# Blocks and token sums split in the order of their use, a third token sum on VectorE, and TensorE's waits moved into the first F pair

## The chip, the cores and the metric

One Trainium2 chip; the program runs on one of its cores. The metric is the device time of one execution in microseconds, the median of several runs. TensorE, VectorE (DVE in the profile), ScalarE (ACT), GpSimd (POOL) and SyncE (SP, which issues the DMAs here) each work through a list of instructions of their own and wait for one another by semaphores.

## The reference

Three stages: a sparse attention (2 batches of 8 heads, 768 tokens, head size 64), a mixture of 4 experts that every token passes, and a routed mixture of 8 experts. The change lies in the second one:

```python
def _moe_ref(x, domain_probs, w1, w2):      # x: 1536 x 512
    p = domain_probs / (domain_probs.sum(-1, keepdims=True) + 1e-09)
    out = np.zeros((N, D), dtype=np.float32)
    for e in range(4):                      # w1: 512 x 1024, w2: 1024 x 512
        h = np.maximum(x @ w1[e], 0.0)
        out += p[:, e:e + 1] * (h @ w2[e])
    return out
```

## The kernel before

**High and low parts.** A float32 product is made of three matmuls on a high part (rounded by ScalarE) and a low part (the rest, subtracted by VectorE): high x high, high x low, low x high. So each weight and each activation is split before TensorE can use it: ScalarE writes `..._hi`, then VectorE writes `..._lo`.

**The order of the mixture.** Expert 0 runs for all four groups of 384 tokens along with the attention (`group_steps`, c = 0 to 3). Then come five *passes* (`PASSES`): experts 1, 2, 3 on batch 0, then experts 1 and 2 on batch 1; pass 3 (`SWITCH`) is the first of batch 1. Expert 3 on batch 1 is done after them in the plain way, as c = 4 and 5 of `group_steps` (c = G is the first of these two).

**A pass.** Its first layer (`factors`) is a block multiplication in seven products instead of eight. w1 is cut into 2 x 2 blocks; three of them are used as they are (A11, A12, A22), the fourth arrives in the place of S4 and is overwritten by it. S1 to S4 are sums of blocks, T1 to T4 sums of the halves of x. For each of four F pairs i TensorE makes the products in the order A12, S1·T1, A11, A22·T4, S2·T2, S4, S3·T3, six matmuls of 128x384 each (`block`, lines 2000 to 2002). ScalarE takes products out of PSUM (`put`), VectorE adds a second product to them (`join`, line 1362), and both split the result into `hb_hi` and `hb_lo`. The second layer (`rows_out`) makes six row tiles of 24 matmuls of 128x512 on PSUM banks 2 and 3 in turn; VectorE adds each to `acc` (`add_more`, line 1377), and row tile tt waits for the addition of tile tt - 2. For expert 0 that addition is `add_rows`, line 1224.

**The preparation of the next pass.** SyncE loads four blocks (`load_blocks`) when the pass before has made its last product. VectorE makes S1 to S4 in place (`block_sums`, lines 1336 to 1344), ScalarE rounds all seven blocks in `BLOCK_ORDER` (`high_blocks`, line 953), VectorE makes the low parts (`low_blocks`, line 1350, 128x1024 each). VectorE does this between the additions of the row tiles. When the batch changes (before pass 0 and before pass 3) the token sums come too: T1, T2 and T4 on VectorE (lines 1308 to 1324, three, two and two subtractions or additions of 128x768), T3 on GpSimd (`third_sum`, lines 758 to 762); ScalarE rounds them (`high_sums`, line 964), VectorE makes their low parts (`low_sums`, line 1329). Before pass 3 SyncE brings back the half of x that was set aside (`x_back`).

**What TensorE waits for.** Ahead of a pass it waits for all seven low blocks of the pass and, in passes 0 and 3, for all four low sums:

```python
pe.wait_ge(acc_ok, 2 + GR * G)
for t in range(len(PASSES)):
    pe.wait_ge(block_ok, BLOCKS * (t + 1))
    if t in (0, SWITCH):
        pe.wait_ge(t_ok, 4 * (PASSES[t][0] + 1))
    factors(t, route_fill if t == SWITCH else lambda k: None)
```

The wait for `acc_ok` stands ahead of the loop and is for the last addition of expert 0. After the last pass TensorE waits for `rows_added` of all 30 row tiles and, in c = G, for all four low pieces of w1 (`w1_ok`), of which VectorE makes the last one (`low_w1`, line 1206) after the last row addition. During pass 3 TensorE also transposes finished rows for the router (`route_turn`, line 1939), which wait for `rows_added` of the first three passes.

Of the kernel before, what the change touches and what calls it, by code (L numbers as in the profile page):

```python
# [18 lines left out]
def sparse_attention_moe_moe(nc, q, k, v, dprobs, w1, w2, w_skip, w_gate, v1, v2, out):  # L19
# [60 lines left out]
    BLOCK_ORDER = (A22, A11, S1, A12, S3, S2, S4)  # L80
    T1, T2, T3, T4 = range(4)
    T_ORDER = (T1, T2, T4, T3)
# [36 lines left out]
    with ExitStack() as ctx:  # L119
# [296 lines left out]
        def _(sp):  # L416
# [251 lines left out]
        def _(gp):  # L668
# [80 lines left out]
            def third_sum(b):  # L749

                (b12, b12_lo), (b22, b22_lo) = x_block(0, 1), x_block(1, 1)
                to = halves(t_sum_at(b, T3))
                if b:
                    gp.wait_ge(x_back, 32)
                else:
                    gp.wait_ge(x_saved, 32)
                    gp.wait_ge(l1_done, FC * G)
                nc.gpsimd.tensor_tensor(to, b22, b12, ALU.subtract).then_inc(t_pool, 1)
                gp.wait_ge(t_pool, 3 * b + 1)
                nc.gpsimd.tensor_tensor(to, to, b22_lo, ALU.add).then_inc(t_pool, 1)  # L760
                gp.wait_ge(t_pool, 3 * b + 2)
                nc.gpsimd.tensor_tensor(to, to, b12_lo, ALU.subtract).then_inc(t_pool, 1)

            for b in range(B):
                third_sum(b)

# [56 lines left out]
        def _(act):  # L823
# [121 lines left out]

            def high_blocks(t):

                for k, j in enumerate(BLOCK_ORDER):
                    if j in (A22, A11, A12):
                        act.wait_ge(block_sent[(A22, S4, A11, A12).index(j)], 16 * (t + 1))  # L950
                    else:
                        act.wait_ge(block_sum, 4 * t + (S1, S3, S2, S4).index(j) + 1)
                    nc.scalar.activation(block_part(wb_hi, j), block_in(j), ACT.Copy).then_inc(block_hi_ok, 1)

            def high_sums(b):

                for k, j in enumerate(T_ORDER):
                    if j == T3:
                        act.wait_ge(t_pool, 3 * (b + 1))
                    else:  # L960
# [1284 lines left out]
```

## Time and profile before

| | |
|---|---|
| median of 3 runs | 753.19 us (750.95 to 754.45) |
| the profiled execution's own time | 749.69 us |
| its span | 748.0 us |
| TensorE busy | 711.6 us (95%) |
| TensorE weight loads | 587.3 us (79%) |
| VectorE busy | 430.7 us (58%) |
| ScalarE busy | 291.5 us (39%) |
| GpSimd busy | 83.7 us (11%) |
| TensorE's mean granted clock | 0.990 |

Times in the profile count from the first instruction of the span. Matmuls overlap, so a matmul's duration is longer than the distance from its start to the next one's, and a group's busy time says less about TensorE than its pauses. A wait for several semaphores is put down to the one that came last. In the chain of waits each piece begins where the piece before it ended; a run of the same instruction is one piece (x3, x4).

### The profile page before, as it was taken

The numbers are of one execution on the slowest core, as the hardware profiler recorded it, in microseconds if no ns is written. First come the engines' busy times: TensorE is split into PE (matmuls) and PEld (weight loads), VectorE is DVE, ScalarE is ACT, GpSimd is POOL, SyncE is SP. The second block draws the span as 40 slices with busy tenths as digits, with TensorE's granted clock in tenths as the row PEclk, the third lists the DMA queues.
The fourth block names the chain that finished last, engine by engine and source line by source line (L and its number), as shares of the span: only waits on it lengthen the run. The fifth ranks groups of instructions, "written<-read, shape, count | busy, mean of one in ns | idle before, by whom it ended". The sixth has DMA issues, their size and how long they took to land.

```text
span 748.0 us, 12356 instructions
## 1 busy us (share of the span) xinstructions
PE 711.6 (95%) x4530; PEld 587.3 (79%) x4531; DVE 430.7 (58%) x1055; ACT 291.5 (39%) x651; POOL 83.7 (11%) x103
## 2 busy tenths in 40 slices
PE   5699999999979999999997899999989999999997
PEld 4588898988869889989985898899888986444454
DVE  4987665453976745773769459756543154544341
ACT  4654454451516605533641356055122211533330
POOL 2611000000400000000012000200000003432321
PEclk9999999999999999999999999999999999999999
DMA  9894722213423303303070733033215269599900
GB/s 205 214 207 91 155 61 56 51 28 95 186 85 112 113 1 114 109 4 113 3 279 1 253 113 113 1 113 113 84 60 195 85 222 373 202 398 395 391 18 21
DMA packets 88239, 101.60 MB, mean 136 GB/s; under 512 B 54616, under 2 KB 54892, under 8 KB 87280
## 3 DMA queue, kind: packets, MB, share of 16 engines
q1 hardware_dynamic: 85520, 96.14, 40.0%
q0 software_dynamic: 2656, 4.66, 2.0%
q8 instruction: 35, 0.57, 0.3%
q14 instruction: 28, 0.23, 0.1%
HBM read 88.32 MB, written 12.96 MB: 135 GB/s over the span
## 4 chain that ended last, share of the span: by engine, by line
PE 77%; DVE 13%; DMA 6%; issue 2%; SPq 1%; ACT 1%; POOL 0%; DVEq 0%; POOLq 0%
PE ps L1757 14%; PE ps L1759 13%; PE ps L1758 13%; PE ps L2000 7%; PE ps L2001 6%; PE ps L2002 6%; PE ps L2153 4%; PE ps L2125 4%; DMA sets<-in_moe_w 3%; DVE wb_lo L1350 3%; DMA xt_lo<-x_aside 2%; PE ps L1819 2%; PE ps L1791 2%; PE ps L1950 1%; PE ps L1805 1%
## 5 line engine op out<-in xcount | busy, mean ns | idle before, releaser
L2000 PE MATMUL ps<-xt_hi,wb_hi 128*128 128x384 f32 x280 | 94.7, 338 | 6.0 <-DVE acc L1224 3.9
L2002 PE MATMUL ps<-xt_hi,wb_lo 128*128 128x384 f32 x280 | 94.3, 337 | 0.0
L2001 PE MATMUL ps<-xt_lo,wb_hi 128*128 128x384 f32 x280 | 94.3, 337 | 0.0
L969 ACT ACTIVATE h_raw<-ps 128x384 f32<-128x384 f32 x80 | 39.3, 491 | 105.8 <-PE ps L2002 103.8
L1758 PE MATMUL ps<-v_lo_acc,hb_hi 128*128 128x512 f32 x180 | 70.6, 392 | 0.0
L1757 PE MATMUL ps<-xt_hi,w_hi 128*128 128x384 f32 x188 | 65.6, 349 | 2.4 <-issue 2.1
L1362 DVE TENSOR_TENSOR h_raw<-ps,h_raw 128x384 f32<-128x384 f32 x80 | 41.3, 552 | 42.9 <-PE ps L2002 42.9
L1759 PE MATMUL ps<-xt_hi,w_lo 128*128 128x384 f32 x188 | 63.1, 336 | 0.0
L1758 PE MATMUL ps<-xt_lo,w_hi 128*128 128x384 f32 x188 | 63.0, 335 | 0.0
L907 ACT ACTIVATE h_hi<-ps 128x384 fp32r<-128x384 f32 x48 | 23.6, 492 | 97.1 <-PE ps L1759 96.9
L1757 PE MATMUL ps<-w_hi,h_hi 128*128 128x512 f32 x144 | 58.2, 404 | 0.4 <-DVE acc L1224 0.4
L2000 PEld LDWEIGHTS ps<-xt_hi,wb_hi 128*128 128x128 f32 x280 | 53.1, 190 | 6.9 <-issue 6.8
L975 ACT ACTIVATE hb_hi<-h_raw 128x384 fp32r<-128x384 f32 x80 | 40.8, 525 | 43.2 <-DVE h_raw L1362 43.1
L1759 PE MATMUL ps<-w_hi,h_lo 128*128 128x512 f32 x144 | 56.4, 391 | 0.0
L1758 PE MATMUL ps<-w_lo,h_hi 128*128 128x512 f32 x144 | 56.2, 390 | 0.0
L2001 PEld LDWEIGHTS ps<-xt_lo,wb_hi 128*128 128x128 f32 x280 | 53.0, 189 | 0.1
L2125 PE MATMUL ps<-sets,acc 128*64 128x512 f32 x224 | 51.6, 599 | 1.6 <-DVE sets L1698 0.6
L2002 PEld LDWEIGHTS ps<-xt_hi,wb_lo 128*128 128x128 f32 x280 | 53.1, 189 | 0.0
L1757 PE MATMUL ps<-v_hi_first,hb_hi 128*128 128x512 f32 x120 | 47.6, 396 | 5.1 <-DVE acc L1377 5.1
L2153 PE MATMUL ps<-sets,acc 128*64 128x256 f32 x448 | 51.6, 382 | 0.7 <-ACT acc L1059 0.7
L1377 DVE SCALAR_TENSOR_TENSOR acc<-ps,dp,acc 128x512 f32<-128x512 f32 x30 | 22.5, 749 | 48.4 <-PE ps L1759 48.4
L1367 DVE SCALAR_TENSOR_TENSOR hb_lo<-h_raw,hb_hi 128x384 fp32r<-128x384 f32 x80 | 42.1, 554 | 12.0 <-ACT hb_hi L975 11.8
(262 smaller groups left out, 1400.1 us busy)
## 6 DMA issues: line engine op xcount, KB each, us to landing
sets<-in_moe_w SPq DMA_DIRECT2D x72, 512.0 KB, 7.8
w_raw<-in_moe_w SPq DMA_DIRECT2D x20, 512.0 KB, 6.1
acc<-in_moe_w SPq DMA_DIRECT2D x10, 768.0 KB, 5.3
stage<-in_moe_w SPq DMA_DIRECT2D x8, 512.0 KB, 4.5
stage<-in_k SPq DMA_DIRECT2D x16, 192.0 KB, 4.7
acc<-in_v SPq DMA_DIRECT2D x4, 768.0 KB, 6.4
x_rows<-acc SPq DMA_DIRECT2D x4, 768.0 KB, 6.0
out_rows<-acc SPq DMA_DIRECT2D x4, 768.0 KB, 7.6
```

The source lines that it names most:

```text
L969: nc.scalar.activation(h_raw[:, f, half * GT:(half + 1) * GT], ps[:, bank, 0:GT], ACT.Copy).then_inc(put_by, 1)
L975: nc.scalar.activation(hb_hi[cols], h_raw[cols], ACT.Relu).then_inc(hb_hi_ok, 1)
L1362: TT(to, ps[:, bank, 0:GT], to, ALU.add).then_inc(joined, 1)
L1367: nc.vector.scalar_tensor_tensor(out=hb_lo[cols], in0=h_raw[cols], scalar=0.0, in1=hb_hi[cols].bitcast(F32), op0=ALU.max, op1=ALU.subtract ...
L1757: mm(dst, a_hi, b_hi, start=start, stop=False)
L1758: mm(dst, a_hi, b_lo, start=False, stop=False)
L1759: return mm(dst, a_lo, b_hi, start=False, stop=stop)
L2000: mm(to, wb_hi[w], hi(c), start=(c == 0 and not onto), stop=False, skip_group_check=onto)
L2001: mm(to, wb_hi[w], lo(c), start=False, stop=False, skip_group_check=onto)
L2002: last = mm(to, wb_lo[w], hi(c), start=False, stop=(c == HALF_D - 1), skip_group_check=onto)
L2125: last = mm(ps[j * QT:(j + 1) * QT, 0, 0:FQ], xt2[:, from_c:from_c + QT], wset[:, 0, at:at + FQ], start=(c == 0), stop=(c == KC - 1))
L2153: last = mm(ps[j * QT:(j + 1) * QT, bank, 0:DQ], ht2[:, at:at + QT], wset[:, 0, to:to + DQ], start=(f == 0), stop=(f == FC - 1))
```

## The change

`BLOCK_ORDER` and `T_ORDER` become the order in which the products use them, and the split of a token sum follows that of the block it is used with (`T_AFTER`), on ScalarE, on VectorE and in TensorE's waits. SyncE loads the four blocks in another order. The wait for the low parts goes from ahead of the pass into `block`, where each of the seven products of the first F pair waits for its own. `third_sum` moves from GpSimd to VectorE: before pass 0 it stands ahead of the low blocks, before pass 3 after row tile 3's addition. Between the row tiles of pass 2, VectorE's work is put in a new order (`between`); in pass 3 the last four low blocks go behind the fifth addition. In c = G the first product is made as all high-weight matmuls, then the low ones, each waiting for its piece, and the wait for `rows_added` goes behind the first layer.

```diff
-    BLOCK_ORDER = (A22, A11, S1, A12, S3, S2, S4)
+    BLOCK_ORDER = (A12, S1, A11, A22, S2, S4, S3)
...
-    T_ORDER = (T1, T2, T4, T3)
+    T_ORDER = (T1, T4, T2, T3)
+    T_AFTER = {S1: T1, A22: T4, S2: T2, S3: T3}
...
-                for k, (to, row, col) in enumerate(((A22, 1, 1), (S4, 0, 1), (A11, 0, 0), (A12, 1, 0))):
+                for k, (to, row, col) in enumerate(((A12, 1, 0), (S4, 0, 1), (A22, 1, 1), (A11, 0, 0))):
...
             def high_blocks(t):
+                for j in BLOCK_ORDER:
+                    high_block(t, j)
+                    if t in (0, SWITCH) and j in T_AFTER:
+                        high_sum(PASSES[t][0], T_AFTER[j])
...
+            def third_sum(b):
+                (b12, b12_lo), (b22, b22_lo) = x_block(0, 1), x_block(1, 1)
+                to = halves(t_sum_at(b, T3))
+                if b == 0:
+                    dve.wait_ge(x_saved, 32)
+                    dve.wait_ge(l1_done, FC * G)
+                follow(TT(to, b22, b12, ALU.subtract))
+                follow(TT(to, to, b22_lo, ALU.add))
+                TT(to, to, b12_lo, ALU.subtract).then_inc(t_sum, 1)
...
-            low_blocks(0, range(3))
+            third_sum(0)
+            low_blocks(0, range(2))
             add_rows(c, 0, c, 0, True)
-            low_blocks(0, range(3, BLOCKS))
+            low_blocks(0, range(2, 4))
             add_rows(c, 0, c, 1, True)
-            low_sums(0)
+            low_blocks(0, range(4, BLOCKS))
             add_rows(c, 0, c, 2, True)
...
+                if t + 1 == SWITCH:
+                    if tt == 0:
+                        block_sums(t + 1, 0)
+                        block_sums(t + 1, 1)
+                    if tt == 1:
+                        low_blocks(t + 1, range(1))
+                    if tt == 2:
+                        first_sum(1)
+                        second_sum(1)
+                    if tt == 3:
+                        fourth_sum(1)
+                        third_sum(1)
+                    if tt == 4:
+                        low_blocks(t + 1, range(1, 4))
+                    if tt == 5:
+                        low_blocks(t + 1, range(4, BLOCKS))
+                    return
...
+                elif c == G:
+
+                    pe.wait_ge(joined, 4 * FP * len(PASSES))
+                    pe.wait_ge(h_ok, FC * c + 1)
+                    for kc in range(KC):
+                        pe.wait_ge(w1_hi_ok, PIECES * e + kc + 1)
+                        mm(ps[:, 0, 0:GT], w1_hi[:, kc, 0:P], xt_hi[:, kc, 0:GT], start=(kc == 0), stop=False)
+                        mm(ps[:, 0, 0:GT], w1_hi[:, kc, 0:P], xt_lo[:, kc, 0:GT], start=False, stop=False)
+                    for kc in range(KC):
+                        pe.wait_ge(w1_ok, PIECES * e + kc + 1)
+                        last = mm(ps[:, 0, 0:GT], w1_lo[:, kc, 0:P], xt_hi[:, kc, 0:GT], start=False, stop=(kc == KC - 1))
...
+                if c == G:
+                    pe.wait_ge(rows_added, TPH * len(PASSES))
...
-            def block(j, i, moving, bank, onto=False):
+            def block(t, j, i, moving, bank, onto=False):
 
                 hi, lo = moving
+                if i == 0:
+                    pe.wait_ge(block_ok, BLOCKS * t + BLOCK_ORDER.index(j) + 1)
+                    if t in (0, SWITCH) and j in T_AFTER:
+                        pe.wait_ge(t_ok, 4 * PASSES[t][0] + T_ORDER.index(T_AFTER[j]) + 1)
...
             for t in range(len(PASSES)):
-                pe.wait_ge(block_ok, BLOCKS * (t + 1))
-                if t in (0, SWITCH):
-                    pe.wait_ge(t_ok, 4 * (PASSES[t][0] + 1))
                 factors(t, route_fill if t == SWITCH else lambda k: None)
...
-            pe.wait_ge(rows_added, TPH * len(PASSES))
```

The change moves instructions at three places. First VectorE in front of pass 0, from the low blocks to the last addition of expert 0 (`wb_lo` is a low block, `xt_lo` a low token sum, `acc` a row addition). Before:

```order
L1350 TENSOR_TENSOR wb_lo<-w_raw,wb_hi 128x1024 [waits block_hi_ok] x3
L1224 TENSOR_SCALAR acc<-ps,dp 128x512 [waits l2_done]
L1350 TENSOR_TENSOR wb_lo<-w_raw,wb_hi 128x1024 [waits block_hi_ok] x4
L1224 TENSOR_SCALAR acc<-ps,dp 128x512 [waits l2_done]
L1329 TENSOR_TENSOR xt_lo<-t_raw,xt_hi 128x768 [waits t_hi_ok] x2
L1329 TENSOR_TENSOR xt_lo<-h_rows,xt_hi 128x768 [waits t_hi_ok]
L1329 TENSOR_TENSOR xt_lo<-x_raw,xt_hi 128x768 [waits t_hi_ok]
L1224 TENSOR_SCALAR acc<-ps,dp 128x512 [waits l2_done]
```

With the change, whose lines are those of the changed program, from the last step of the third sum (`x_raw`) on:

```order
L1316 TENSOR_TENSOR x_raw<-x_raw,xt_lo 128x768 [waits t_step]
L1341 TENSOR_TENSOR wb_lo<-w_raw,wb_hi 128x1024 [waits block_hi_ok] x2
L1320 TENSOR_TENSOR xt_lo<-t_raw,xt_hi 128x768 [waits t_hi_ok]
L1206 TENSOR_SCALAR acc<-ps,dp 128x512 [waits l2_done]
L1341 TENSOR_TENSOR wb_lo<-w_raw,wb_hi 128x1024 [waits block_hi_ok] x2
L1320 TENSOR_TENSOR xt_lo<-h_rows,xt_hi 128x768 [waits t_hi_ok]
L1206 TENSOR_SCALAR acc<-ps,dp 128x512 [waits l2_done]
L1341 TENSOR_TENSOR wb_lo<-w_raw,wb_hi 128x1024 [waits block_hi_ok]
L1320 TENSOR_TENSOR xt_lo<-t_raw,xt_hi 128x768 [waits t_hi_ok]
L1341 TENSOR_TENSOR wb_lo<-w_raw,wb_hi 128x1024 [waits block_hi_ok] x2
L1320 TENSOR_TENSOR xt_lo<-x_raw,xt_hi 128x768 [waits t_hi_ok]
L1206 TENSOR_SCALAR acc<-ps,dp 128x512 [waits l2_done]
```

Each low sum follows the block it is used with, and the first two additions stand behind fewer low blocks; the last addition is still the last of the list.

Second VectorE at the switch, from the fourth token sum's last step to the first join of pass 3 (`h_raw`). Before:

```order
L1324 TENSOR_TENSOR x_raw<-x_raw,xt_lo 128x768 [waits t_step]
L1350 TENSOR_TENSOR wb_lo<-w_raw,wb_hi 128x1024 [waits block_hi_ok] x3
L1377 SCALAR_TENSOR_TENSOR acc<-ps,dp,acc 128x512 [waits rows_done]
L1350 TENSOR_TENSOR wb_lo<-w_raw,wb_hi 128x1024 [waits block_hi_ok] x4
L1377 SCALAR_TENSOR_TENSOR acc<-ps,dp,acc 128x512 [waits rows_done]
L1329 TENSOR_TENSOR xt_lo<-x_raw,xt_hi 128x768 [waits t_hi_ok] x4
L1377 SCALAR_TENSOR_TENSOR acc<-ps,dp,acc 128x512 [waits rows_done]
L1362 TENSOR_TENSOR h_raw<-ps,h_raw 128x384 [waits put_by,product]
```

With the change, from the third token sum's last step on, which now follows the fourth sum:

```order
L1316 TENSOR_TENSOR x_raw<-x_raw,xt_lo 128x768 [waits t_step]
L1370 SCALAR_TENSOR_TENSOR acc<-ps,dp,acc 128x512 [waits rows_done]
L1341 TENSOR_TENSOR wb_lo<-w_raw,wb_hi 128x1024 [waits block_hi_ok]
L1320 TENSOR_TENSOR xt_lo<-x_raw,xt_hi 128x768 [waits t_hi_ok]
L1341 TENSOR_TENSOR wb_lo<-w_raw,wb_hi 128x1024 [waits block_hi_ok] x2
L1320 TENSOR_TENSOR xt_lo<-x_raw,xt_hi 128x768 [waits t_hi_ok]
L1370 SCALAR_TENSOR_TENSOR acc<-ps,dp,acc 128x512 [waits rows_done]
L1341 TENSOR_TENSOR wb_lo<-w_raw,wb_hi 128x1024 [waits block_hi_ok]
L1320 TENSOR_TENSOR xt_lo<-x_raw,xt_hi 128x768 [waits t_hi_ok]
L1341 TENSOR_TENSOR wb_lo<-w_raw,wb_hi 128x1024 [waits block_hi_ok] x2
L1320 TENSOR_TENSOR xt_lo<-x_raw,xt_hi 128x768 [waits t_hi_ok]
L1355 TENSOR_TENSOR h_raw<-ps,h_raw 128x384 [waits put_by,product]
```

Three low blocks and two low sums now stand behind the last addition, and the first join behind them. Ahead of this piece, row tile 2's addition now stands before the first token sum instead of after the second.

Third TensorE at the start of pass 0: the last matmul of expert 0 and the first products. Before:

```order
L1759 MATMUL ps<-w_hi,h_lo 128x512
L2000 MATMUL ps<-xt_hi,wb_hi 128x384 [waits h_ok,acc_ok,pt_ready,block_ok,o_lo,t_ok,s_const,wg_in]
L2001 MATMUL ps<-xt_lo,wb_hi 128x384
L2002 MATMUL ps<-xt_hi,wb_lo 128x384
L2000 MATMUL ps<-xt_hi,wb_hi 128x384
```

With the change:

```order
L1763 MATMUL ps<-w_hi,h_lo 128x512
L2023 MATMUL ps<-xt_hi,wb_hi 128x384 [waits h_ok,pt_ready,acc_ok,o_lo,block_ok,s_const,wg_in]
L2024 MATMUL ps<-xt_lo,wb_hi 128x384
L2025 MATMUL ps<-xt_hi,wb_lo 128x384
L2023 MATMUL ps<-xt_hi,wb_hi 128x384
L2024 MATMUL ps<-xt_lo,wb_hi 128x384
L2025 MATMUL ps<-xt_hi,wb_lo 128x384
L2023 MATMUL ps<-xt_hi,wb_hi 128x384 [waits t_ok,block_ok]
```

The first product's wait for the low sums (`t_ok`) has gone to the second, `block_ok` is asked for by each; `acc_ok` has stayed with the first.

## Rows read from the trace of the kernel before

**Rows 1.** Waits of TensorE from 180 to 600 us: who for, total, times, longest.
```profile
PE ps L1757 <- DVE acc L1377: 5.1, 1, 5.1
...
PE ps L2000 <- DVE acc L1224: 3.9, 1, 3.9
...
PE ps L2000 <- DVE xt_lo L1329: 2.1, 1, 2.1
...
PE ps L1757 <- issue: 2.1, 1, 2.1
...
PE ps L1757 <- DVE acc L1224: 0.4, 1, 0.4
```

**Rows 2.** The chain of waits before pass 0: start us, us, what.
```profile
196.89 1.14 DVE w_raw L1341
...
198.13 2.70 DVE w_raw L1344
...
201.29 6.26 DVE wb_lo L1350 x3
...
216.88 0.67 DVE acc L1224
```

**Rows 3.** The chain of waits between pass 2 and pass 3.
```profile
390.44 2.49 DVE x_raw L1309
...
405.50 4.54 DVE wb_lo L1350 x4
...
410.04 0.66 DVE acc L1377
...
410.70 3.48 DVE xt_lo L1329 x4
```

**Rows 4.** TensorE's timeline: start us, us, line, operation, out<-in.
```profile
405.22 0.39 PE L1757 MATMUL ps<-v_hi_first,hb_hi 128*128 128x512 f32 x1
...
411.35 0.40 PE L1757 MATMUL ps<-v_hi_last,hb_hi 128*128 128x512 f32 x1
...
414.32 0.41 PE L2000 MATMUL ps<-xt_hi,wb_hi 128*128 128x384 f32 x1 [2.11 <-DVE xt_lo L1329]
...
417.53 0.34 PE L2001 MATMUL ps<-xt_lo,wb_hi 128*128 128x384 f32 x1
...
419.44 0.33 PE L2000 MATMUL ps<-xt_hi,wb_hi 128*128 128x384 f32 x1
...
550.41 0.41 PE L1757 MATMUL ps<-xt_hi,w_hi 128*128 128x384 f32 x1 [2.10 <-issue]
```

**Rows 5.** VectorE's timeline, in brackets the idle time before and its releaser.
```profile
389.44 0.96 DVE L1308 TENSOR_TENSOR x_raw<-xt_hi 128x768 f32<-128x768 f32 x1 [4.19 <-DMA xt_lo<-x_aside]
...
418.60 0.56 DVE L1362 TENSOR_TENSOR h_raw<-ps,h_raw 128x384 f32<-128x384 f32 x1 [3.76 <-PE ps L2002]
...
549.09 1.22 DVE L1206 TENSOR_TENSOR w_lo<-stage,w_hi 128x1024 fp32r<-128x1024 f32 x1
```

**Rows 6.** Windows: busy time and count per engine, granted clock (PEclk), DMA.
```profile
217.90:221.80 3.90, 3.90 (x14) 3.90 (x15) 0.08 (x1) 0.49 (x1) 0.00 (x0) 0.56 0.87 320
...
399.60:402.40 2.80, 2.77 (x7) 2.19 (x8) 2.77 (x3) 1.12 (x3) 0.00 (x0) 0.50 0.02 6
...
414.30:418.00 3.70, 3.68 (x24) 3.67 (x25) 0.53 (x1) 1.82 (x4) 0.00 (x0) 1.00 0.87 288
```

**Rows 7.** Groups of VectorE from 185 to 218 us: busy, mean ns, idle before.
```profile
L1309 DVE TENSOR_TENSOR t_raw<-t_raw,xt_lo 128x768 f32<-128x768 f32 x1 | 1.0, 957 | 0.0
```

**Rows 8.** GpSimd's timeline before pass 0.
```profile
197.10 2.63 POOL L758 TENSOR_TENSOR x_raw<-xt_hi 128x768 f32<-128x768 f32 x1 [35.63 <-PE ps L1759]
```

**Rows 9.** Timeline of SyncE's queue and of ScalarE in pass 3.
```profile
430.16 0.91 SPq L537 DMA_DIRECT2D acc<-in_moe_w  x2
...
442.71 0.62 ACT L983 ACTIVATE v_hi_first<-acc 128x512 fp32r<-128x512 f32 x1
```

**Rows 10.** The chain of waits in the tail.
```profile
650.55 11.20 DMA sets<-in_moe_w
```

More of the change, by code:

```diff
@@ L747, in _ @@
             nc.gpsimd.iota(place_no[:, :], pattern=[[0, SIDES], [1, QT]], base=-int(FAR), channel_multiplier=0, allow_small_or_imprecise_dtypes=True).then_inc(place_made, 1)
[L749 to L765, printed above, removed]
             def send_entries(g):
@@ L1555, in _, with between @@
             link(nc.vector.tensor_scalar_add(side_first[:, :], side[:, :], float(-SIDES)))
+            def between(t, tt):
+                if t + 1 == SWITCH:
[15 more added lines that the diff above has]
+                    return
+                if t + 1 < len(PASSES):
+                    if tt == 0:
+                        block_sums(t + 1, 0)
+                        block_sums(t + 1, 1)
+                    if tt == 1:
+                        low_blocks(t + 1, range(3))
+                    if tt == 2 and t < SWITCH:
+                        low_blocks(t + 1, range(3, BLOCKS))
+                    if tt == 4 and t >= SWITCH:
+                        low_blocks(t + 1, range(3, BLOCKS))
+                elif tt == 1:
+                    low_w1(1, lambda j: stage[:, j, :], [0, 1, 2])
+                if t >= SWITCH:
+                    if tt == 0:
+                        choose(t - SWITCH)
+                    if tt == 2:
+                        places(t - SWITCH)
+                    if tt == 3:
+                        enter(t - SWITCH)
+                    if tt == 4:
+                        early_sum(t - SWITCH)
@@ L1574, in _ @@
-                add_more(t, 2)
-                if t + 1 == SWITCH:
-                    fourth_sum(1)
-                    low_blocks(t + 1, range(3))
-                if t >= SWITCH:
-                    places(t - SWITCH)
-                elif t + 1 < SWITCH:
-                    low_blocks(t + 1, range(3, BLOCKS))
-                add_more(t, 3)
-                if t >= SWITCH:
-                    enter(t - SWITCH)
-                if more and t + 1 >= SWITCH:
-                    low_blocks(t + 1, range(3, BLOCKS))
@@ L1587, in _ @@
-                add_more(t, 4)
-                if t + 1 == SWITCH:
-                    low_sums(1)
-                if t >= SWITCH:
-                    early_sum(t - SWITCH)
-                add_more(t, 5)
+                for tt in range(TPH):
+                    add_more(t, tt)
+                    between(t, tt)
             dve.wait_ge(rows_done, TPH * len(PASSES))
@@ L1873, in group_steps @@
                     yield
+                elif c == G:
[8 more added lines that the diff above has]
+                        last = mm(ps[:, 0, 0:GT], w1_lo[:, kc, 0:P], xt_hi[:, kc, 0:GT], start=False, stop=(kc == KC - 1))
+                    last.then_inc(l1_done, 1)
+                    yield
                 else:
                     pe.wait_ge(w1_ok, PIECES * e + PIECES)
-                for f in range(1 if first and c == 0 else 0, FC):
+                for f in range(1 if c in (0, G) else 0, FC):
                     pe.wait_ge(h_ok, FC * c + f + 1)
```

77 lines of the change are left out of this document (28 added, 49 removed).

## The prediction

> **What bounds the kernel now.** TensorE does, and the first view to read is the list of what it waited for [rows 1]. Seven pauses stand between the last attention step and the last layer; five of them, 5.1, 3.9, 2.1, 2.1 and 0.4 us, are the ones that the change can reach. They lie at three places. (a) Before pass 0 the tail of layer 2 is done at 214.0 (the pause of 3.9 before the matmul at 217.90); the 0.4 is a little earlier, before the third row tile. (b) Between pass 2 and pass 3, where the batch changes, TensorE stands for 5.1 us before row tile 4 and for 2.1 before pass 3. (c) Before the last mixture group it stands for 2.1.
>
> The chain of waits says what was late at (a) and (b): VectorE without a break, the low parts of blocks and token sums and the row additions between them [rows 2, 3]. At (c) it is one row addition and then one low part of w1, 549.09 to 550.31, and TensorE starts at 550.41 [rows 4, 5]. The windows show a second price: after the pauses of 3.9 and 5.1 us the granted clock is 0.56 and 0.50 (the 1.2 GHz level) for some 3.9 and 2.8 us, after that of 2.1 it is 1.00 (2.4 GHz) [rows 6]. So 3.9 us cost a further 3.9 x 0.44 = 1.7, and 5.1 us a further 1.7: row tiles 4 and 5 run from 399.6 to 412.2, 12.6 us, where 2 x 24 matmuls at (411.35 - 405.22) / 27 = 0.227 us make 10.9 [rows 4].
>
> **GpSimd's third sum.** It looks free, but VectorE pays for it. The same subtraction of 128x768 takes 0.96 us while GpSimd rests [rows 7] and 2.49 beside GpSimd's third sum [rows 3]; that happens three times at the switch (2.49, 2.49, 2.46), 4.55 us too many. Before pass 0 GpSimd starts at 197.10 [rows 8], the fourth block sum takes 2.70 instead of 1.14 to 1.24 (1.5 too many) and three low blocks 6.26 where four take 4.54 elsewhere, that is 3.41 for three (2.85 too many) [rows 2, 3]: 4.3 us. In VectorE's hands a third sum is three dependent subtractions at just under 1.00 us from start to start (389.44 to 390.44 [rows 3, 5]), the last a little less, 2.85 us. Net VectorE gains 4.3 - 2.85 = 1.5 us before pass 0 and 4.55 - 2.85 = 1.7 at the switch.
> The Trainium skill (Perfetto Trace Analysis, Optimizing Scalar/DVE Operations) speaks against the move: where VectorE is saturated, work may be handed to GpSimd, and here it comes back. By that rule alone, with nothing given back, both third sums would be pure cost and the sum below would end near 751.7 us instead of 741.0 (VectorE's list 2.85 longer before pass 0 and 4.55 longer at the switch than the sum has it). The rows take the other side, since they show the give-back of 4.3 and 4.55 us.
>
> **(a) Before pass 0.** The waits for blocks and sums go into the first F pair, but the wait for the last row addition (acc_ok) stays ahead of the first block, and that addition stands on VectorE behind all seven low blocks and all four low sums, before and after. So splitting the wait brings nothing here; pass 0 still starts when VectorE's whole list is done. The list is 1.5 us shorter: the addition ends at 217.55 - 1.5 = 216.1, TensorE starts 0.35 later as now, at 216.4. The 0.4 pause goes too (the first addition now stands behind two low blocks and a sum, not three slow blocks, and ends near 206.5, before the 207.9 at which TensorE asks), so TensorE's pause becomes 216.4 - 213.6 = 2.8 us. Which clock follows? 2.8 is nearer to 2.1 (full clock) than to 3.9 (half), so I take the full clock: 1.7 us more, with 0 and 1.7 as bounds. **Gain 1.5 + 1.7 = 3.2 us.**
>
> **(b) The switch.** The restored half of x lands at 389.44, VectorE having idled 4.19 us for it [rows 5]; in that idle time go the first low block (4.54 / 4 = 1.14) and the block sums, which now wait for the third and fourth transfer instead of the second and third. Row tile 2's addition now stands ahead of the token sums, done by 389.8, so tile 4 starts at 394.5 without a pause and tile 5 at 400.0; rows end at 394.5 + 10.9 = 405.4, against 412.2. Then VectorE, from 389.8 without idling: sums 3 + 2 + 2 + 3 subtractions, 2.85 + 1.86 + 1.86 + 2.85 = 9.4; three additions of 0.66; six low blocks of 1.14 = 6.8; four low sums of 3.48 / 4 = 0.87 [rows 3]. Together 21.7, so it is through at 411.5. Block by block TensorE is served: A12 was ready at 388, S1 with T1 at 402.7, A11 403.8, A22 with T4 405.8, the sixth addition 406.5 (the first transposes ask for it near 407.5). What is late next is not a block: S2 waits for the **join** of A11's product, and on VectorE the first join stands behind the three last low blocks and two low sums. S2 would come 419.44 - 414.32 = 5.1 us after the pass's start [rows 4], at 410.5; the join (0.56, [rows 5]) ends at 411.5 + 0.8 = 412.3. A new pause of about 1.9 us. S2 starts at 412.4 instead of 419.44. **Gain 7.0 us.** Bounds: 8.9 if no join is late, 5 if VectorE is 2 us later than summed.
>
> **(c) The last group.** TensorE no longer waits for the sixth addition and all of w1's low parts; it starts at 548.3 with eight matmuls of high w1 at (419.44 - 417.53) / 11 = 0.174 us [rows 4], 1.4 in all, and three low ones (to 550.2); the fourth needs the low part that ends at 550.31, unchanged. f = 0 ends near 550.6 instead of 552.6. **Gain 1.95 us**, bounds 1.0 and 2.1.
>
> **Costed at nothing.** The extra waits: 7 x 5 first-pair blocks and 8 in the last group, 43 matmuls. The matmul at 419.44 also waits for satisfied semaphores and runs 0.33 us like its neighbours, the one after a real pause 0.41 [rows 4]; so 0 is taken, and 43 x 0.08 = 3.4 us is the upper bound. In pass 3 four low blocks move behind the fifth addition; VectorE otherwise idles before the sixth, and the blocks concerned are the last four to be asked for. Second-layer weights of pass 3 are requested at 430.16 [rows 9], ACT first needs them at 442.71; their request hangs on the sixth addition (some 8 us earlier) and lands in time although the pass is 7 us earlier. ScalarE's seven blocks and four sums are the same work; at the switch it waits for sums, ahead of VectorE each time.
>
> **The sum.** 3.2 + 7.0 + 1.95 = 12.15 us. The profiled execution took 749.69 us (span 748.0 and 1.7 around it), so 737.5 in its terms. It stands 3.5 below the median of the runs, 753.19; the gain is taken off that: **741.0 us**.
>
> **Rivals.**
> 1. The half clock stays after the 2.8 us pause: 1.7 less, 742.7. For it: both longer pauses had it; against: the one of 2.1 before pass 3 had not [rows 6]. 0.13.
> 2. The waits cost TensorE: 3.4 us, 744.4. Against it, the row at 419.44. 0.12. The Trainium skill (Perfetto Trace Analysis, Identifying Dependency Chains) says that an instruction which waits on several engines may get EventSemaphore instructions ahead of it, and Advanced Engine Details and Errata (Network/Comms) puts reading a semaphore at 50 to 100 ns: an estimate from those pages is 2.2 to 4.3 us. No run here shows that price.
> 3. The gain comes back in the tail, where transfers of expert weights (one of 11.2 us [rows 10]) are on the chain. Against: each is issued behind an event of the streams that move earlier. If so, about 750. 0.04.
> 4. Slower than before: the slow subtractions are not GpSimd's doing but belong to their operands, and stay; the third sum then costs VectorE 3 x 2.49 = 7.5 us at both places. Pass 0 would start at 217.55 + 7.5 = 225.0, 7.1 later; at the switch VectorE's list would be 4.55 + 4.65 longer, S2 at 421.6, 2.1 later; less 1.95 at the end: 7.3, so 760.5. It decides from about 1.9 us per subtraction on. Against: [rows 7], the same shape at 0.96 with GpSimd at rest. 0.03. The milder case, old ones slow and the third sum fast, is the 751.7 above: 0.02. The Trainium skill (SBUF — State Buffer, Who interferes with whom) has a VectorE instruction with two SBUF inputs blocked by a GpSimd one that reads SBUF, for its whole length; by that rule, with which the trace agrees (2.49 against 0.96), rival 4 falls.
> The forecast itself: 0.66.
>
> **The numbers.** About 0.5% (3.8 us) is what a measurement can tell from no change. Faster by more: forecast, rivals 1 and 2, 0.91. Within: rival 3 and the 751.7 case, 0.06. Slower: 0.03. The range: 738 (no late join, and the scatter of runs, about 1.7 us to either side) to 746 (rival 2 with scatter).
>
> **What would show it.** Right: no GpSimd subtraction; no VectorE subtraction over 1.3 us; a pause of about 2.8 us before pass 0 that ends with acc's addition, at full clock after it; none before tiles 4 and pass 3; one of about 1.9 us inside pass 3's first pair before S2, ended by VectorE's h_raw; under 0.3 us before the last w1_lo matmul. Wrong: slow subtractions without GpSimd, a pass 0 that starts before its last addition, no pause at S2, spacings over 0.174 us at the new waits, or new waits in the tail.

## The result and the profile after

| | before | after |
|---|---|---|
| median of the runs, us | 752.67 (750.95 to 754.45) | 739.13 (737.58 to 741.88) |
| ratio to before | 1 | 0.9835 [0.9806, 0.9863] |
| profiled execution, us | 749.69 | 737.88 |
| its span, us, and mean granted clock | 748.0, 0.990 | 736.1, 0.998 |

The changed kernel takes 1.65% less. The forecast was 741.0 us in a range of 738 to 746. The same kernel was run twice more beside the experiments: 740.94 us, ratio 0.9853 [0.9826, 0.988], and 740.06 us, ratio 0.9855 [0.9829, 0.988]. Against the median that the prediction started from, 753.19, the forecast is a ratio of 0.984.

The page of the changed kernel, its span, the busy time of each engine and the chain that ended last:

```profile
span 736.1 us, 12384 instructions
...
PE 707.5 (96%) x4530; PEld 583.7 (79%) x4531; DVE 427.6 (58%) x1061; ACT 291.6 (40%) x651; POOL 68.1 (9%) x97
...
PE 78%; DVE 12%; DMA 5%; issue 2%; SPq 1%; ACT 1%; POOL 0%; POOLq 0%; DVEq 0%; ACTq 0%
```

What TensorE waited for from 180 to 600 us, to be held against [rows 1]:

```profile
PE ps L2023 <- DVE acc L1206: 3.0, 1, 3.0
PE ps L2023 <- DVE h_raw L1355: 1.7, 1, 1.7
PE ps L1761 <- DVE h_lo L1197: 0.3, 1, 0.3
PE ps L1761 <- DVE v_lo_end L1348: 0.3, 1, 0.3
```

Seven pauses have become four. The two that count are the one before pass 0, still ended by acc's last addition, and one that before did not have: it stands inside pass 3 and is ended by `h_raw`, VectorE's join. TensorE's timeline shows where they stand, and the start of the last group (all rows of line 1884 and 1885 up to 539.16 are 0.17 to 0.19 us apart):

```profile
216.44 0.41 PE L2023 MATMUL ps<-xt_hi,wb_hi 128*128 128x384 f32 x1 [3.02 <-DVE acc L1206]
...
409.18 0.45 PE L2023 MATMUL ps<-xt_hi,wb_hi 128*128 128x384 f32 x1 [1.74 <-DVE h_raw L1355]
...
537.92 0.33 PE L1884 MATMUL ps<-xt_hi,w_hi 128*128 128x384 f32 x1
...
539.33 1.24 PE L1888 MATMUL ps<-xt_hi,w_lo 128*128 128x384 f32 x4
540.41 0.33 PE L1761 MATMUL ps<-xt_hi,w_hi 128*128 128x384 f32 x1
```

VectorE's timeline, first the third token sum and the last addition before pass 0, then the third sum and the end of the list at the switch:

```profile
199.85 0.95 DVE L1314 TENSOR_TENSOR x_raw<-xt_hi 128x768 f32<-128x768 f32 x1
200.84 0.96 DVE L1315 TENSOR_TENSOR x_raw<-x_raw,xt_lo 128x768 f32<-128x768 f32 x1
201.83 0.96 DVE L1316 TENSOR_TENSOR x_raw<-x_raw,xt_lo 128x768 f32<-128x768 f32 x1
...
215.44 0.74 DVE L1206 TENSOR_SCALAR acc<-ps,dp 128x512 f32<-128x512 f32 x1
...
386.72 0.95 DVE L1290 TENSOR_TENSOR x_raw<-xt_hi 128x768 f32<-128x768 f32 x1
...
396.05 0.96 DVE L1316 TENSOR_TENSOR x_raw<-x_raw,xt_lo 128x768 f32<-128x768 f32 x1
...
405.43 2.36 DVE L1341 TENSOR_TENSOR wb_lo<-w_raw,wb_hi 128x1024 fp32r<-128x1024 f32 x2
407.70 0.96 DVE L1320 TENSOR_TENSOR xt_lo<-x_raw,xt_hi 128x768 fp32r<-128x768 f32 x1
408.57 0.56 DVE L1355 TENSOR_TENSOR h_raw<-ps,h_raw 128x384 f32<-128x384 f32 x1
```

No subtraction takes 2.49 us any more [rows 3]; all ten steps of the four sums at the switch, 386.72 to 396.05, take 0.95 or 0.96. The join at 408.57 follows the last low sum without a gap: TensorE waits for VectorE's list, not for the product. And the windows, in the columns of [rows 6]:

```profile
216.40:220.00 3.60, 3.56 (x21) 3.59 (x22) 0.29 (x3) 0.99 (x2) 0.00 (x0) 1.00 0.81 303
...
409.20:412.80 3.60, 3.60 (x26) 3.60 (x26) 1.12 (x2) 1.36 (x3) 0.00 (x0) 1.00 1.05 408
```

In this execution both stretches after the pauses run at 1.00, the 2.4 GHz level. Both kernels have a pause of 0.33 us in front of 188 us, which serves as a mark in all that follows; it ends at 188.34 before and at 188.45 after, so the times of the two profiles can be compared to about 0.1 us. Pass 0 starts 1.46 us earlier, 216.44 against 217.90. S2 of pass 3 starts 10.26 earlier, 409.18 against 419.44: 1.46 from before pass 0, 1.6 that the half clock no longer takes there (the request for pass 3's blocks on SyncE's queue is already 3.02 earlier, 369.65 against 372.67), and 7.2 at the switch. The last group adds 1.9: its second layer-1 product starts 12.19 earlier, 540.41 against 552.60. The end of the span is 11.9 earlier, so the tail took back 0.3.

### The profile page after: what moved, and what is told of

It is laid out like the page before. It is cut to its first block, busy times and chain, and to the rows that moved or that the text cites. A ratio compares the mean times of both kernels' runs of the same rounds, so it can differ in the third digit from the quotient of the medians.

```text
span 736.1 us, 12384 instructions
## 1 busy us (share of the span) xinstructions
PE 707.5 (96%) x4530; PEld 583.7 (79%) x4531; DVE 427.6 (58%) x1061; ACT 291.6 (40%) x651; POOL 68.1 (9%) x97
## 4 chain that ended last, share of the span: by engine, by line
PE 78%; DVE 12%; DMA 5%; issue 2%; SPq 1%; ACT 1%; POOL 0%; POOLq 0%; DVEq 0%; ACTq 0%
PE ps L1761 14%; PE ps L1763 14%; PE ps L1762 14%; PE ps L2023 6%; PE ps L2025 6%; PE ps L2024 6%; PE ps L2172 4%; PE ps L2144 4%; DMA sets<-in_moe_w 3%; DVE wb_lo L1341 2%; PE ps L1823 1%; PE ps L1795 1%; PE ps L1969 1%; PE ps L1809 1%; DVE xt_lo L1320 1%
## 5 line engine op out<-in xcount | busy, mean ns | idle before, releaser
L960 ACT ACTIVATE hb_hi<-h_raw 128x384 fp32r<-128x384 f32 x80 | 40.9, 526 | 45.3 <-DVE h_raw L1355 45.2
L1360 DVE SCALAR_TENSOR_TENSOR hb_lo<-h_raw,hb_hi 128x384 fp32r<-128x384 f32 x80 | 42.2, 555 | 12.0 <-ACT hb_hi L960 11.9
L1197 DVE SCALAR_TENSOR_TENSOR h_lo<-ps,h_hi 128x384 fp32r<-128x384 f32 x48 | 26.6, 555 | 37.3 <-ACT h_hi L890 37.2
```

The costliest lines, as they stand in the source:

```text
L960: nc.scalar.activation(hb_hi[cols], h_raw[cols], ACT.Relu).then_inc(hb_hi_ok, 1)
L1360: nc.vector.scalar_tensor_tensor(out=hb_lo[cols], in0=h_raw[cols], scalar=0.0, in1=hb_hi[cols].bitcast(F32), op0=ALU.max, op1=ALU.subtract ...
```

## The experiments

All ratios are to the kernel before on the same chip. The changed kernel's own ratio stands at 0.9835, 0.9853 and 0.9855 in its three series; one thousandth is 0.75 us. Where only the place of a pause is asked, the profile answers more sharply than the ratio.

### What each part is worth

**The third sum alone** (`third_alone`): the kernel before, with `third_sum` in VectorE's hands and everything else as it was.

```diff
-                nc.gpsimd.tensor_tensor(to, b22, b12, ALU.subtract).then_inc(t_pool, 1)
...
+                follow(TT(to, b22, b12, ALU.subtract))
+                follow(TT(to, to, b22_lo, ALU.add))
+                TT(to, to, b12_lo, ALU.subtract).then_inc(t_sum, 1)
```

> The kernel before with nothing changed but the third token sum, which VectorE makes ahead of the first low block and, at the switch, after the fourth sum. My theory (GpSimd's subtractions block VectorE's): no VectorE subtraction of 128x768 over 1.0 us, pass 0 starts 1.5 us earlier (pause near 2.7), row tile 4 after a pause of some 0.5 instead of 5.1, but row tile 5 now waits some 3 us, since its addition stands behind both last sums and three low blocks, and pass 3 starts 1.9 us earlier than before. Gain 3.4 to 5.0 us, by the clock after the pause before pass 0: 748 to 749.5. Rival (the slow subtractions belong to their operands): slower than before by some 7 us.

Measured: 747.92 us (745.42 to 750.15), just under the range expected, ratio 0.9951 [0.9934, 0.9969]. TensorE's waits from 180 to 600 us that are over 0.35 us:

```profile
PE ps L1991 <- DVE acc L1203: 3.1, 1, 3.1
PE ps L1748 <- DVE acc L1366: 3.0, 1, 3.0
PE ps L1748 <- issue: 2.1, 1, 2.1
PE ps L1991 <- DVE xt_lo L1318: 1.4, 1, 1.4
```

Handing VectorE more work made the kernel 0.5% faster. The old subtractions, which took 2.49, take what they take while GpSimd rests; VectorE's timeline of this kernel:

```profile
390.58 0.96 DVE L1295 TENSOR_TENSOR x_raw<-xt_hi,x_raw 128x768 f32<-128x768 f32 x1
```

Rival 4 and its milder case are gone. The net price is the one that was summed. From the mark to the start of expert 0's last addition it is 28.46 us before (188.34 to 216.80) and 26.97 here (188.90 to 215.87), 1.5 less; at the switch, from the start of the first sum to that of the sixth addition, 24.65 before (389.44 to 414.09) and 22.96 here (387.60 to 410.56), 1.7 less.

**The third sum back on GpSimd** (`third_back`): the changed kernel with GpSimd's `third_sum` again, the rest as changed (the same lines as above, the other way round).

> The changed kernel with the third sum back on GpSimd, all else as changed. My theory: VectorE's slow subtractions return, 4.3 us before pass 0 and 4.5 at the switch against 2.85 us of work saved at each, so pass 0 starts at 217.9 (pause near 4.4, then the 1.2 GHz level, 1.6 us more) and the join before S2 is 1.7 later: 743 to 744 against 739.1. Rival (the third sum on VectorE is pure cost, as the rule on handing work over would have it): 2.85 less at both places, 733 to 736.

Measured: 744.04 us (743.58 to 748.75), ratio 0.9922 [0.9895, 0.9949]. The two pauses have grown to 4.1 and 2.4 us, both still ended by the same instructions, and from the mark to the last addition it is 28.46 us again (189.37 to 217.83). The timelines of GpSimd and of VectorE beside it at the switch:

```profile
391.54 2.44 POOL L761 TENSOR_TENSOR x_raw<-x_raw,xt_lo 128x768 f32<-128x768 f32 x1
394.06 2.44 POOL L763 TENSOR_TENSOR x_raw<-x_raw,xt_lo 128x768 f32<-128x768 f32 x1
...
392.32 2.48 DVE L1312 TENSOR_TENSOR x_raw<-x_raw,xt_lo 128x768 f32<-128x768 f32 x1
394.83 2.49 DVE L1313 TENSOR_TENSOR x_raw<-x_raw,xt_lo 128x768 f32<-128x768 f32 x1
397.35 0.96 DVE L1319 TENSOR_TENSOR x_raw<-xt_hi,x_raw 128x768 f32<-128x768 f32 x1
```

The same form takes 2.49 and, one instruction later, 0.96. The rows also show what the 2.49 is made of. GpSimd's steps end at 393.98 and 396.50, VectorE's two subtractions at 394.80 and 397.32, each 0.82 us after the GpSimd step that was running when it began; in the kernel before, all three slow ones at the switch end 0.81 after such a step, and the first one there, which began at 389.44, ahead of GpSimd's first step at 389.49, took 0.96. So VectorE's instruction is not slowed by a factor: it ends some 0.8 us after GpSimd's does. Before pass 0 GpSimd's three steps stand at 198.26, 200.83 and 203.63, and VectorE's two low blocks in that time take 5.20 where the next two take 2.34. So the slowness comes and goes with GpSimd's own subtraction and with nothing else that was varied. The Trainium skill (SBUF — State Buffer, Who interferes with whom) has a VectorE instruction with two inputs in SBUF held up by one of GpSimd that reads SBUF; the trace agrees, 2.49 against 0.96. On handing a saturated VectorE's work to GpSimd, the Trainium skill (Perfetto Trace Analysis, Optimizing Scalar/DVE Operations) says that it may make sense, and in its next sentence that the two share a port for reading SBUF, so that it might not help; the prediction told only the first half and took it for a rule against the move. The runs side with the second half, in both directions: taking the work back gained 0.5%, giving it away again cost about 0.7%.

**The waits ahead of the pass** (`waits_whole`): the changed kernel, whose new orders stay, but TensorE waits for all blocks and sums before each pass.

```diff
-                if i == 0:
-                    pe.wait_ge(block_ok, BLOCKS * t + BLOCK_ORDER.index(j) + 1)
...
+                pe.wait_ge(block_ok, BLOCKS * (t + 1))
+                if t in (0, SWITCH):
+                    pe.wait_ge(t_ok, 4 * (PASSES[t][0] + 1))
```

> The changed kernel, but TensorE waits for all seven low blocks and all four low sums ahead of the pass as before; the orders stay as changed. My theory: pass 0 and passes 1, 2, 4 start as now; pass 3 starts when the last low sum is there, near 408.8 instead of 402.7, a pause of over 6 us with the 1.2 GHz level behind it, and no pause before S2; S2 4.7 us later and 1.6 for the clock: 743.8 to 745.4. Rival (splitting the waits is worth nothing, the orders do it all): 739. Rival (the split waits cost TensorE): pass for pass the F pairs are shorter here than in the changed kernel.

Measured: 746.57 us (745.11 to 747.15), ratio 0.9937 [0.9919, 0.9955], a little over what was expected.

```profile
PE ps L2019 <- DVE xt_lo L1320: 6.4, 1, 6.4
PE ps L2019 <- DVE acc L1206: 3.1, 1, 3.1
```

The pause before pass 0 is nearly as it was (3.1 for 3.0), so splitting the wait buys nothing there, as the prediction had it: acc's addition is what counts. At the switch it buys the difference of 6.4 and 1.7, and in this profile the long pause was followed by the half clock as well (409.30 to 413.30 at 0.50). Both were in the expectation, and the profiled execution, 745.11 us, lies within it. That the median is above 745.4 comes at least in part from where the expectation was counted: from the 739.1 of the first series. From 740.2, the median of all 16 executions of the changed kernel, the same 4.7 and 1.6 give 746.5.

**The last group undone** (`end_undone`): the changed kernel with the old start of the last mixture group.

```diff
-                    for kc in range(KC):
-                        pe.wait_ge(w1_ok, PIECES * e + kc + 1)
...
+            pe.wait_ge(rows_added, TPH * len(PASSES))
```

> The changed kernel with the last group's start as before: waits for all row additions and all four low pieces of w1 ahead of it. My theory: the pause of 2.1 us before the last group is back, 741.0 against 739.1. Rival (the tail had slack of its own): 739.

Measured: 743.57 us (739.04 to 744.65), ratio 0.9878 [0.9851, 0.9906]. The pause of 2.10 us is back (540.21 to 542.31). The median is 2.6 us above the expectation, which was counted from 739.1 too; by the ratios (0.9878 against 0.985) the loss is about 2 us, the pause itself. In the profile the pause is followed by a stretch at half clock that the same pause before did not have:

```profile
542.30:546.30 4.00, 3.99 (x14) 4.00 (x15) 0.00 (x0) 0.07 (x1) 0.00 (x0) 0.57 0.43 131
```

One execution took 739.04, the others 740.37 to 744.65; the mean granted clock was 0.999 in the fastest and 0.990 to 0.995 in the others. Whether the clock makes this pause dearer in most executions is not shown.

### What a wait that is already met costs

**More waits** (`more_waits`): the waits in all four F pairs, ahead of 105 more products, 24 of which wait for a token sum as well.

```diff
-                if i == 0:
+                if True:
```

> The changed kernel with the waits for blocks and sums in all four F pairs of every pass instead of the first alone: 105 more waits of TensorE, each for something that is there long before. My theory: a wait that is already met costs nothing that can be seen, so 739 to 741 us as the changed kernel, the first matmul of every block 0.17 to 0.18 us behind the last of the block before. The rival of the prediction, in which a met wait costs TensorE the gap of a matmul restarted behind a wait (0.08 us, what a pause of the trace lacks at the least): 105 x 0.08 = 8.4 us more, 747 to 749.

Measured: 739.98 us (739.22 to 742.63), ratio 0.9858 [0.9836, 0.9879], against 740.06 of the changed kernel beside it. Nothing was added, and 105 x 0.08 = 8.4 us were at stake; the pauses are again 3.0 and 1.7. The first and the last of 42 matmuls in the later F pairs of pass 0, six to a product:

```profile
228.76 0.33 PE L2024 MATMUL ps<-xt_lo,wb_hi 128*128 128x384 f32 x1
...
235.87 0.33 PE L2023 MATMUL ps<-xt_hi,wb_hi 128*128 128x384 f32 x1
```

(235.87 - 228.76) / 41 = 0.173 us, the spacing of a stream without new waits: the same 42 in the changed kernel, 228.65 to 235.76, take 7.11 us as well. Rival 2 is wrong. The prediction's estimate of 2.2 to 4.3 us for 43 waits, from the Trainium skill (Perfetto Trace Analysis, Identifying Dependency Chains; Advanced Engine Details and Errata, Network/Comms, which puts the reading of a semaphore at 50 to 100 ns), does not show either: for 105 waits it would be 5.3 to 10.5 us, and 0 was measured. The two intervals together leave room for some 2.5 us over 105 products, that is 0.02 us for one.

### What is late next

**The join first** (`join_first`): in the changed kernel the low halves of S3 and of T3, the last two of the list, go behind the first join of pass 3.

```diff
                     join(n, 1, 3, BX, i, 0)
+                    if t == SWITCH and i == 0:
+                        low_blocks(t, range(6, BLOCKS))
...
-                        low_blocks(t + 1, range(4, BLOCKS))
+                        low_blocks(t + 1, range(4, 6))
```

> The changed kernel, but at the switch the last low block (S3) and the last low sum (T3) stand behind the first join of pass 3. My theory: the join is then ready before S2 is due, the pause of 1.7 us goes: 737.4. Rival (S3's own wait takes its place): a pause before S3 of about the same length, 739.

Measured: 738.83 us (736.95 to 739.57), ratio 0.9829 [0.9803, 0.9856]. All of TensorE's waits over 0.25 us from 180 to 600:

```profile
PE ps L2025 <- DVE acc L1206: 3.0, 1, 3.0
PE ps L1763 <- DVE h_lo L1197: 0.3, 1, 0.3
PE ps L1763 <- DVE v_lo_end L1348: 0.3, 1, 0.3
```

The pause before S2 was VectorE's list in front of the join, and nothing else was late behind it. That is read from the profile; the time alone does not tell this kernel from the changed one beside it (0.9853 [0.9826, 0.988]).

**acc later** (`acc_later`): TensorE waits for acc's last addition not before pass 0 but before pass 0's row tiles, which are the first to need it.

```diff
-            pe.wait_ge(acc_ok, 2 + GR * G)
...
+                if t == 0:
+                    pe.wait_ge(acc_ok, 2 + GR * G)
```

> The changed kernel, but the wait for expert 0's last row addition goes from ahead of pass 0 to ahead of its first row tile. My theory: it alone holds pass 0 back, since A12 and the others are ready in time; the pause of 3.0 us goes, and with it the clock's choice: 3.0 to 4.6 less than the changed kernel, 735 to 736. Rival (the low parts of blocks and sums, or the first join behind them, hold TensorE as well): a new pause of 1 us or more in pass 0's first pair, gain under 2.

Measured: 737.37 us (736.13 to 741.76), ratio 0.9819 [0.9787, 0.9851], less than hoped. By the ratio it is some 2.6 us less than the changed kernel beside it, and the intervals overlap. The pause of 3.0 is gone, and one of 1.7 that was not expected has come, 15 us later, ahead of the last product of pass 0's second F pair (it ends at 229.93; pass 0 starts at 214.51):

```profile
PE ps L2023 <- DVE h_raw L1355: 1.8, 1, 1.8
PE ps L2023 <- ACT h_raw L954: 1.7, 1, 1.7
```

ScalarE's timeline says why. It had to make `v_hi_first` and stood for the data; `h_raw`, for which TensorE waited, was behind it in ScalarE's queue:

```profile
228.07 0.63 ACT L968 ACTIVATE v_hi_first<-acc 128x512 fp32r<-128x512 f32 x1 [3.49 <-DMA acc<-in_moe_w]
228.61 0.51 ACT L960 ACTIVATE hb_hi<-h_raw 128x384 fp32r<-128x384 f32 x1
229.02 0.85 ACT L954 ACTIVATE h_raw<-ps 128x384 f32<-128x384 f32 x2
```

And SyncE's queue says why the data was late: acc has to be saved before the weights may take its place, and the save waits for the last addition, which ends at 217.4.

```profile
217.46 0.37 SPq L588 DMA_DIRECT2D x_rows<-acc  x1
223.64 0.92 SPq L538 DMA_DIRECT2D acc<-in_moe_w  x2
```

So the early start moved TensorE up to the next thing that hangs on the same addition.

**Both** (`both`): the two edits together.

> Both edits at once. My theory: they add up, 4.7 to 6.3 less than the changed kernel, 733 to 734.5, and TensorE has no pause over 0.5 us between 190 us and the tail. Rival (a later step takes it back, the second-layer weights of pass 3 for one): under 3 us.

Measured: 735.90 us (733.41 to 737.22), ratio 0.9791 [0.9763, 0.9818], clear of the changed kernel's 0.9853 [0.9826, 0.988], and one pause of 1.7, ScalarE's, is left. The median is above the 733 to 734.5 expected, by about this pause; that expectation was made before the pause was known.

**The addition earlier** (`best`): both edits, and in VectorE's list before pass 0 the last addition stands ahead of the last two low halves instead of behind them.

```diff
-            low_blocks(0, range(4, BLOCKS))
+            low_blocks(0, range(4, 6))
             add_rows(c, 0, c, 2, True)
+            low_blocks(0, range(6, BLOCKS))
```

> Both moves (the wait for acc behind the blocks of pass 0's first F pair, and the low halves of S3 and T3 behind the first join of pass 3), and beside them the last addition of the combine's third row set two low halves earlier in VectorE's list before pass 0. If the pause of 1.74 us in the first F pair of pass 0 hangs on acc (saved behind the last addition, fetched again, then v_hi_first), the last addition at 213.5 instead of 215.4 us takes it away: 734 us, 732.5 to 735. If it hangs on ScalarE's own work, the pause stays at 1.7 us and the time at 736.

Measured: 733.07 us (732.43 to 734.71), ratio 0.9757 [0.9741, 0.9773]. TensorE's waits from 180 to 600 us, complete, and ScalarE's row in its timeline:

```profile
PE ps L1961 <- DVE acc L1208: 0.3, 1, 0.3
PE ps L1764 <- DVE h_lo L1197: 0.3, 1, 0.3
PE ps L2010 <- DVE entry L1504: 0.3, 1, 0.3
PE ps L1764 <- DVE v_lo_end L1348: 0.3, 1, 0.3
```

```profile
225.97 0.63 ACT L968 ACTIVATE v_hi_first<-acc 128x512 fp32r<-128x512 f32 x1 [1.09 <-DMA acc<-in_moe_w]
```

The mark before 188 us ends at 190.01 here and at 188.41 in `both`. From it, the addition starts 26.97 us later in `both` (215.38) and 24.99 in `best` (215.00), and ScalarE's wait falls from 3.53 to 1.09 us. The pause hung on acc, and it is gone. (The expectation puts it in the first F pair; it stood in the second.) This version is faster than the changed kernel beside it, whose ratio was 0.9855 [0.9829, 0.988]. No pause over 0.35 us is left between layer 2's tail and the last group.

### The clock

**The pauses filled** (`filled`): the changed kernel; ahead of the two waits TensorE transposes the identity matrix into a PSUM bank that nobody reads then.

```diff
+                    if t == SWITCH and i == 0:
+                        for _ in range(14):
+                            nc.tensor.transpose(ps[:, 4, 0:P], ident[:, :], ident[:, :])
                     pe.wait_ge(joined, 4 * n + 1)
...
+            for _ in range(26):
+                nc.tensor.transpose(ps[:, 4, 0:P], ident[:, :], ident[:, :])
             pe.wait_ge(acc_ok, 2 + GR * G)
```

> The changed kernel with 26 transposes of the identity matrix ahead of the wait for acc before pass 0, and 14 ahead of the wait for the join before S2 in pass 3, into a PSUM bank that nobody reads then. A row of such transposes shows 12 in 1.47 us, so they fill 3.0 and 1.7 us. Theory (the stretches at 1.2 GHz come because TensorE stood idle): no pause of over 0.5 us at either place, granted clock 1.00 from 216 to 224 us and from 407 to 420 us, median 1 to 3 us below the changed kernel and its executions closer together. Rival (the stretches come by execution, whatever TensorE does): the same time as the changed kernel, and the mean granted clock between 0.990 and 0.998 as before. If transposes come late, a pause turns into up to 0.5 us of delay at each place.

**The changed kernel twice more** (`after_again`, `after_third`).

> The changed kernel once more, beside the next three on the same chip: 739 by any theory. The clock: if the pause of 3.0 us before pass 0 is followed by full clock in some executions and by the 1.2 GHz level in others, its times spread over some 2 us or more.

> The changed kernel once more on the same chip as the other three, to compare them with: 739 to 741 us, ratio 0.982 to 0.986.

Measured: `filled` 737.66 us (736.72 to 740.41), ratio 0.9819 [0.9799, 0.9839], mean granted clock 0.995 to 1.000; `after_third` beside it 740.06 (738.24 to 744.94), clock 0.986 to 0.997; `after_again` 740.94 (738.74 to 743.48), clock 0.991 to 0.995. The windows after the first pause, in `after_third` and then in `filled`:

```profile
217.10:221.10 4.00, 3.99 (x14) 4.00 (x15) 0.16 (x2) 0.85 (x2) 0.00 (x0) 0.59 0.85 315
```

```profile
217.10:221.10 4.00, 4.00 (x24) 3.96 (x24) 0.83 (x4) 0.98 (x2) 0.00 (x0) 1.00 0.78 293
```

14 matmuls against 24 in the same 4 us. The transposes add useless work and do no harm: TensorE starts pass 0 when it would have started anyway. By the medians they bring 2.4 us, but the two intervals overlap, so the time alone does not prove it; the profiles do for the place. In `after_again` the stretch came after the pause of 1.73 us too, and lasted:

```profile
215.60:219.40 3.80, 3.64 (x14) 3.67 (x15) 0.31 (x2) 0.61 (x2) 0.00 (x0) 0.63 0.80 294
410.10:412.00 1.90, 1.90 (x9) 1.90 (x10) 0.56 (x1) 1.30 (x3) 0.00 (x0) 0.78 1.04 405
412.00:420.00 8.00, 8.00 (x35) 8.00 (x34) 0.56 (x1) 1.65 (x4) 0.00 (x0) 0.50 0.83 321
```

From S2 to the pause of 0.3 us behind it, the same work takes 40.9 us there (410.07 to 450.96) and 36.1 in the first profile (409.18 to 445.25): 4.8 us for one stretch. In `after_third` no such stretch followed the same pause.

## Why the prediction was right, and where only in part

**(a) Before pass 0.** The list's length was exact: the addition was forecast to end at 216.1 and does at 216.10 (the next instruction's start); TensorE was forecast at 216.4 and starts at 216.44. The pause is 3.0 instead of 2.8 because layer 2's tail, without its 0.4 pause, ends at 213.4. That splitting the wait brings nothing here is shown by `waits_whole`. The step "so I take the full clock" was decided between two values that both occur: at full clock in the profile of the result, at 0.63 and 0.59 in those of the two repeats. So the forecast and rival 1 are not two theories of which one is true; they are two executions of one kernel. In the eight profiles with a pause of 3.0 or 3.1 us before pass 0 the half clock followed in five (`after_again`, `after_third`, `third_alone`, `end_undone`, `more_waits`) and the full clock in three (the result, `waits_whole`, `join_first`). The chance of 0.13 for rival 1 was far too low, and that the profiled execution of the result shows full clock there was luck. The 16 executions of the changed kernel have a median of 740.2 us between 737.6 and 744.9, with mean clocks of 0.998 in the two fastest and 0.986 in the slowest. The term for what follows the pause should have been about half of 1.7, with the other half as scatter.

**(b) The switch.** Gain 7.2 for 7.0, the pause 1.7 for 1.9, at the place named and ended by the instruction named. The halves of x landed early enough in this profile for VectorE to begin the sums at 386.7 without idling for them, and the list was through 21.85 us later (408.57), for 21.7 summed. What was called late next, the join and not a block, is shown by `join_first`: put the join forward, and the pause is gone.

**(c) The last group.** 1.9 for 1.95; there is no pause at 537.92. In `end_undone` the pause came back with its 2.1 us, and the ratio says about 2 us as well.

**Costed at nothing.** The waits: right, and by far, with waits ahead of 105 more products adding nothing. (The prediction's 43 counts products; eight of them, in passes 0 and 3, wait for a token sum as well.) The later low blocks and the earlier request for the second-layer weights: in the first profile TensorE has no pause over 0.35 us between S2 of pass 3 and the last group.

**GpSimd's third sum.** Both halves of the step hold: the give-back (`third_alone`, faster by 0.5% with more work for VectorE) and its size, 1.5 and 1.7 us of VectorE's list net in `third_alone`, as forecast. In TensorE's pauses it is less: `third_back` has them 1.0 and 0.7 us longer. At the switch that is in part because GpSimd's first step there began at 389.62, before VectorE was ready for the sums at 390.54, and held up the first of them only to 1.75 us; the rest was not followed up.

**The sum.** 12.15 us forecast, 11.8 between the two profiled executions, of which 12.2 stand at the three places and 0.3 went in the tail. By medians the gain was 13.5 us in the first series, and about 11 by the ratios of the two repeats (0.0146 x 752). The share of the three parts, as experiments: without the third sum's move the kernel is at 0.992, without the split waits at 0.994, without the last group's edit at 0.988, and with none at 1; the three losses (about 5, 6.5 and 2 us against 0.985) add up to 13.5 against a whole of 11, which the intervals do not tell apart; if the excess is real, the half clock behind the longer pauses of `waits_whole` and `end_undone` is one reason that the profiles offer. What VectorE's new order is worth by itself was not tested: every experiment on the changed kernel keeps it, and `third_alone` has the old order together with the old waits.

**What stays open.** Why a pause is followed by the low level in one execution and not in another. An execution's mean clock does not settle it, since it counts low stretches at other places too: from 18 to 24 us the granted clock is 0.72 in the profiles before and after and 1.00 in that of `after_again`. That `filled` is faster as a time, and not just at full clock in its profile, is likely but not settled.

## What to carry to other kernels

When an engine's waits are split by piece, write out the order of the engine that makes the pieces up to the first thing it must also do inside the consumer's stage (here the join, and then the save of acc); the pause goes there, and its size can be summed from the instructions in front of it. Before moving work to a helper engine, look in the trace for one instruction form beside the helper and without it. Here it took 2.49 us instead of 0.96, and three steps given away cost more of VectorE's time (4.55 us at the switch) than they saved (2.85). A pause of an engine under a clock throttle has a price that differs from execution to execution, so count it as its length and a scatter, and take out the pause rather than hoping for the clock.

## What the runs showed of the hardware that was not expected

- **The half clock after a pause comes and goes with the execution.** Over all profiles of this case (before, after and the twelve experiments), 13 pauses of TensorE of 2.9 to 6.4 us between 180 and 560 us were followed by a stretch at the 1.2 GHz level in 10 cases and not in 3 (the 3.0 of the first profile after, the 3.0 of `join_first`, the 3.1 of `waits_whole`). Of 14 pauses of 1.4 to 2.4 us, 2 were (`after_again` before S2, `end_undone` before the last group). The four kernels without a pause before pass 0 (`acc_later`, `both`, `best`, `filled`) had no such stretch there. Where it was worked out, a stretch cost some 1.6 to 1.7 us; the one of ten microseconds cost 4.8.
- **A wait that is already met costs TensorE nothing that can be seen**: ahead of 105 more products, 739.98 us against 740.06.
- **A VectorE subtraction that begins while GpSimd's is running lasts until 0.8 us after GpSimd's has ended** (128x768 at the switch, 2.49 against 0.96, in the kernel before and in `third_back`). Before pass 0 the 128x1024 forms are held up too: in the kernel before, the fourth block sum ends at 200.83, 1.1 us after GpSimd's step (199.73), and two low blocks of `third_back` took 5.20 against 2.34. A VectorE engine with more to do, but alone, is through earlier.
